# A seven-product (Strassen-Winograd) MLP pair on one core: four PSUM banks per set, P1 copied inside PSUM, sums reordered, Q4 sums on VectorE

## What is computed

```python
def _attn_ref(q, k, v, cap):                 # q, k, v: (2, 12, 448, 64)
    scores = cap * np.tanh(scale * (q @ k.T) / cap)
    attn = softmax(scores)
    return attn @ v
def _moe_ref(x, w_in, w_out):                # x: (896, 768), w_in: (768, 2048), w_out: (2048, 768)
    h = x @ w_in
    r = np.maximum(h, 0.0)
    return (r * r) @ w_out
def _moe2_ref(x, w_in, w_out):
    h = x @ w_in
    return (h / (1.0 + np.exp(-h))) @ w_out
reference = _moe2_ref(_moe_ref(_attn_ref(q, k, v, cap)))
```

## Time and profile before

| | us |
|---|---|
| median of 3 runs | 558.07 |
| the runs | 556.68, 558.07, 2859.89 |
| the profiled execution, its own time | 555.35 |
| its span (first to last instruction) | 553.1 |
| mean granted TensorE clock | 0.989 |

### The profile page before, as it was taken

How to read it: one execution, slowest core, us unless ns; L and a number is a source line. 1 busy time by engine, 2 the same in 40 slices (tenths; PEclk the granted TensorE clock), 3 DMA queues, 4 the chain that set the end, 5 groups by cost and what they waited for, 6 DMA issues and landing times.

```text
span 553.1 us, 7937 instructions
## 1 busy us (share of the span) xinstructions
...
## 2 busy tenths in 40 slices
...
GB/s 230 192 238 239 212 7 66 50 49 80 185 160 169 138 146 125 166 162 148 139 136 138 146 127 62 100 159 192 156 145 147 130 158 156 147 146 143 120 103 101
...
## 3 DMA queue, kind: packets, MB, share of 16 engines
...
...
## 4 chain that ended last, share of the span: by engine, by line
PE 47%; DVE 21%; ACT 15%; issue 8%; DMA 6%; ACTq 0%; DVEq 0%; POOL 0%; POOLq 0%
PE banks L678 12%; PE banks L679 12%; PE banks L680 12%; DVE g_all L1159 5%; ACT g_all L892 4%; PE banks L597 4%; DMA w_q<-w_raw 4%; DVE w_hl L1155 3%; PE banks L590 3%; DVE x_all L1212 2%; ACT work L878 2%; DVE work L1230 2%; ACT w_hl L842 2%; ACT work L885 2%; DVE y L1230 2%
## 5 line engine op out<-in xcount | busy, mean ns | idle before, releaser
L678 PE MATMUL banks<-g_all,w_hl 128*128 128x448 f32 (+1 forms) x339 | 126.3, 373 | 19.5 <-DVE y L1230 7.8
L678 PE MATMUL banks<-x_all,w_hl 128*128 128x448 f32 x342 | 124.9, 365 | 11.7 <-ACT work L859 8.5
L680 PE MATMUL banks<-x_all,w_hl 128*128 128x448 f32 x342 | 124.0, 363 | 0.0
L679 PE MATMUL banks<-g_all,w_hl 128*128 128x448 f32 (+1 forms) x339 | 124.0, 366 | 0.0
L679 PE MATMUL banks<-x_all,w_hl 128*128 128x448 f32 x342 | 123.8, 362 | 0.0
L680 PE MATMUL banks<-g_all,w_hl 128*128 128x448 f32 (+1 forms) x339 | 123.7, 365 | 0.0
L543 POOL DMA_DIRECT2D w_q<-w_raw x64 | 55.4, 973 | 148.2 <-DVE w_hl L1155 127.8
L842 ACT ACTIVATE w_hl<-w_q 128x384 fp32r<-128x384 f32 (+1 forms) x96 | 48.0, 500 | 75.2 <-PE banks L680 38.3
L678 PEld LDWEIGHTS banks<-g_all,w_hl 128*128 128x128 f32 x339 | 64.5, 190 | 34.2 <-issue 12.4
L842 ACT ACTIVATE w_hl<-w_raw 128x384 fp32r<-128x384 f32 (+1 forms) x128 | 63.5, 498 | 41.7 <-PE banks L680 41.4
L543 POOL DMA_DIRECT2D w_raw<-w_raw x32 | 28.5, 890 | 158.1 <-DMA w_raw<-in_moe_w_out_dram 90.6
...
## 6 DMA issues: line engine op xcount, KB each, us to landing
...
```

What stands on the lines that cost most here:

```text
L678: pe.matmul(dst, hi, mov_hi, start=start, stop=False, skip_group_check=onto)
L679: pe.matmul(dst, hi, mov_lo, start=False, stop=False, skip_group_check=onto)
L680: return pe.matmul(dst, lo, mov_hi, start=False, stop=stop, skip_group_check=onto)
```

## The change

The products keep their order. Post-additions are made over four banks A to D. ScalarE copies P1 (product 0) from bank A to bank C (`copy_p1`), where product 3 accumulates to C11. P5 (product 1, bank B) is copied by ScalarE to SBUF (`copy_p5`). VectorE adds bank A after product 2 and P5 into bank D (`make_d`), where product 5 accumulates to C12; product 4 accumulates in A, from which and P5 VectorE makes C22 (`make_22` in PAIR and first-stage GROUP sets; in others `ADD_P5` and `ADD_U3` onto y); product 6 accumulates in A to C21. C11, C12 and C21 of PAIR sets go through `shape` straight from their banks. In first-stage GROUP sets ScalarE copies C11, C12, C21 out; in later ones VectorE adds them to y. T2 and T4 of a PAIR set change tiles (work[0], t_sum). Layer 1's x sums go to work tiles in place of y. Q4 is added by VectorE in all seven-product sets (`add_q4`, before the T sums of the step n=0), and its DMA and the waits for it are gone; SP loads block (0,1) after split 6. The sums and low parts of x chunk 2 move from before set 2 into set 3, and the T1 parts of x to steps 5 and 6 of sets 2 to 4. The last product's two halves use banks A and B of the other half of PSUM. The orders on ScalarE and VectorE are rewritten by hand:

```diff
-    BANK_OF = (0, 1, 0, 2, 0, 1, 0)
-    ONTO = (2, 4, 5, 6)
-
+    BANK_A, BANK_B, BANK_C, BANK_D = range(4)
+    BANK_OF = (BANK_A, BANK_B, BANK_A, BANK_C, BANK_A, BANK_D, BANK_A)
+    ONTO = (2, 3, 4, 5, 6)
...
-               PAIR: (N_B11, N_B22, N_T1, N_T2, N_T3, N_B21, N_T4)}
+               PAIR: (N_B11, N_B22, N_T1, N_T2, N_B21, N_T3, N_T4)}
...
+            eng.wait_ge(s_g, g_no(ahead, {C11: N_T2, C12: N_T3, C22: N_B22, C21: N_B21}[block]))
+            eng.wait_ge(s_t, t_no(ahead, N_T3 if block == C22 else N_T4))
+            if s.kind == PAIR and s.layer == 1 and s.stage == 0 and s.i == 0 and block != C22:
+                eng.wait_ge(s_xo, xo_no(1, KP - 1, {C11: N_T2, C12: N_T3, C21: N_T4}[block]))
+            if block == C22 and sets[s.no - 1].kind == GROUP and sets[s.no - 1].stage > 0:
+                eng.wait_ge(s_take, take_no[sets[s.no - 1].no, ADD_P5])
...
-                    free = {(0, 0): 1, 0: 2, (0, 1): 4, (1, 0): 5, 1: 6, (1, 1): 7}
+                    free = {(0, 0): 1, 0: 2, (0, 1): 6 if q4_by_vector(ahead) else 4, (1, 0): 5, 1: 6, (1, 1): 7}
...
-                add_q4(ahead)
+                if not q4_by_vector(ahead):
+                    add_q4(ahead)
...
+                if n in (2, 3):
+                    pe.wait_ge(s_copy, copy_no[s.no, COPY_P1])
+                elif n in (4, 5):
+                    pe.wait_ge(s_take, take_no[s.no, MAKE_D])
                 else:
-                    pe.wait_ge(s_take, take_no[s.no, of])
+                    pe.wait_ge(s_take, take_no[s.no, MAKE_22 if MAKE_22 in taken_by_vector(s) else ADD_U3])
...
+                elif n == 5 and q4_by_vector(s):
+                    act.wait_ge(s_q4_v, q4_no(s))
...
+            def copy_p1(s):
+                act.wait_ge(s_prod, s.first + 1)
+                act.activation(bank(s, BANK_C), bank(s, BANK_A), ACT.Copy).then_inc(s_copy, 1)
+
+            def copy_p5(s):
+                act.wait_ge(s_prod, s.first + 2)
+                if s.kind == PAIR or s.stage > 0:
+                    work_free(act, s, C22)
+                elif s.layer == 0:
+                    act.wait_ge(s_xo, xo_no(0, s.i, N_T4))
+                act.activation(p5_tile(s), bank(s, BANK_B), ACT.Copy).then_inc(s_copy, 1)
...
+                elif block == C22:
+                    act.wait_ge(s_take, take_no[s.no, MAKE_22])
+                    src = acc(s, C22)
                     scale = -1.0
                 else:
-                    act.wait_ge(s_take, take_no[s.no, 3 + block])
-                    scale = -1.0 if block == C22 else 1.0
+                    n, bank_n = {C11: (3, BANK_C), C12: (5, BANK_D), C21: (6, BANK_A)}[block]
+                    act.wait_ge(s_prod, s.first + n + 1)
+                    src = bank(s, bank_n)
+                    scale = -1.0 if block == C21 else 1.0
+                if s.kind == PLAIN or block != C22:
+                    work_free(act, s, block)
...
-                    if n == 0 and 6 in copied_by_scalar(ahead):
-                        copy(ahead, 6)
+                    if n == 0 and ahead.kind == GROUP and ahead.stage == 0:
+                        copy_out(ahead, COPY_U4)
                     if n == 0 and ahead.kind == PAIR:
                         shape(ahead, C21)
...
-                    if n == 1 and 0 in copied_by_scalar(s):
-                        copy(s, 0)
-                    if n == 3 and 1 in copied_by_scalar(s):
-                        copy(s, 1)
-                        copy(s, 2)
-
-                    if n + 3 < NP:
+                    if n == 1:
+                        copy_p1(s)
+                    if n == 2:
+                        copy_p5(s)
+                    if n == 4 and first_out:
+                        copy_out(s, COPY_C)
+                    if n == 4 and s.kind == PAIR:
+                        shape(s, C11)
+                        square(s, C11)
+                    if n == 6 and first_out:
+                        copy_out(s, COPY_D)
+                    if n == 6 and s.kind == PAIR:
+                        shape(s, C12)
+                        square(s, C12)
+
+                    if n == 2 and q4_by_vector(s) or n < 2:
                         prod_high(s, n + 3)
-                    elif after:
-                        prod_high(after, n + 3 - NP)
-
-                    if s.kind == PAIR and n == 4:
-                        shape(s, C11)
+                    if n == 3 and q4_by_vector(s):
+                        prod_high(s, 6)
+                    if n == 4 and not q4_by_vector(s):
+                        prod_high(s, 6)
+                    if n >= 4 and after:
+                        prod_high(after, n - 4)
+
                     if s.kind == PAIR and n == 5:
-                        square(s, C11)
+                        g_high(s, N_B11)
                         shape(s, C22)
-                        g_high(s, N_B11)
+                        square(s, C22)
                     if s.kind == PAIR and n == 6:
-                        square(s, C22)
-                        shape(s, C12)
                         g_high(s, N_B22)
-                        square(s, C12)
...
                             g_high(ahead, N_T2)
+                            g_high(ahead, N_B21)
+                        if n == 2:
                             g_high(ahead, N_T3)
+                        if n == 3:
+                            g_high(ahead, N_T4)
...
                 if n == N_T1:
-                    wait(dve, s_t, 4 * s.pair)
+                    wait(dve, s_g, NP * s.pair)
+                    if s.layer == 1 and s.stage == 0 and s.i == 0:
+                        dve.wait_ge(s_xo, xo_no(1, KP - 1, N_T1))
                     dve.wait_ge(s_z, max(z_no(s, C11), z_no(s, C12)))
                     made = dve.tensor_tensor(t_sum[:, :], work[0][:, :], work[1][:, :], ALU.subtract)
                 elif n == N_T2:
                     dve.wait_ge(s_t, t_no(s, N_T1))
-                    dve.wait_ge(s_g, g_no(s, N_T1))
+                    dve.wait_ge(s_g, g_no(s, N_B11))
                     dve.wait_ge(s_z, z_no(s, C22))
-                    made = minus_both(t_sum[:, :], t_sum[:, :], work[3][:, :])
+                    made = minus_both(work[0][:, :], t_sum[:, :], work[3][:, :])
                 elif n == N_T3:
                     dve.wait_ge(s_t, t_no(s, N_T1))
                     dve.wait_ge(s_z, z_no(s, C22))
                     made = dve.tensor_tensor(work[1][:, :], work[3][:, :], work[1][:, :], ALU.subtract)
                 else:
                     dve.wait_ge(s_t, t_no(s, N_T2))
-                    dve.wait_ge(s_g, g_no(s, N_B21))
-                    made = minus_both(work[2][:, :], t_sum[:, :], work[2][:, :])
+                    dve.wait_ge(s_g, g_no(s, N_T1))
+                    dve.wait_ge(s_z, z_no(s, C21))
+                    made = minus_both(t_sum[:, :], work[0][:, :], work[2][:, :])
                 made.then_inc(s_t, 1)
...
+                else:
+                    dve.wait_ge(s_xo, xo_no(1, kk - 1, n))
+                if n == N_T1:
+                    dve.wait_ge(s_take, take_no[group.no, ADD_D])
+                    made = dve.tensor_tensor(t_sum[:, :], b11, b12, ALU.subtract)
+                elif n == N_T2:
+                    dve.wait_ge(s_xt, xt_no(1, kk, N_T1))
+                    made = minus_both(work[0][:, :], t_sum[:, :], b22)
+                elif n == N_T3:
+                    made = dve.tensor_tensor(work[1][:, :], b22, b12, ALU.subtract)
+                else:
+                    dve.wait_ge(s_xt, xt_no(1, kk, N_T2))
+                    dve.wait_ge(s_take, take_no[group.no, ADD_U4])
+                    made = minus_both(work[2][:, :], work[0][:, :], b21)
+                made.then_inc(s_xt, 1)
+
...
+            def add_q4(s):
+                dve.wait_ge(s_raw[s.no % 2][1], loads_of(s))
+                dve.wait_ge(s_w_lo, s.first + 3)
+                dve.tensor_tensor(q_block(s, 1), q_block(s, 1), raw_block(s, 0, 1), ALU.add).then_inc(s_q4_v, 1)
+
+            def make_d(s):
+
+                dve.wait_ge(s_prod, s.first + 3)
+                dve.wait_ge(s_copy, copy_no[s.no, COPY_P5])
+                dve.tensor_tensor(bank(s, BANK_D), bank(s, BANK_A), p5_tile(s), ALU.add).then_inc(s_take, 1)
+
+            def make_22(s):
+
+                dve.wait_ge(s_prod, s.first + 5)
+                dve.wait_ge(s_take, take_no[s.no, MAKE_D])
+                if s.kind == PAIR:
+                    dve.tensor_tensor(p5_tile(s), p5_tile(s), bank(s, BANK_A), ALU.add).then_inc(s_take, 1)
+                else:
+                    minus_both(p5_tile(s), p5_tile(s), bank(s, BANK_A)).then_inc(s_take, 1)
...
+            def add_out(s, what):
+
+                n, block, bank_n = {ADD_C: (3, C11, BANK_C), ADD_P5: (1, C22, None), ADD_U3: (4, C22, BANK_A),
+                                    ADD_D: (5, C12, BANK_D), ADD_U4: (6, C21, BANK_A),
+                                    LAST_U3: (4, C21, BANK_A)}[what]
```

(70 more changed lines are left out.)

259 lines of the change are left out of this document (126 added, 133 removed).

## The result

| kernel | runs | median us | lowest to highest | ratio to before, 95% interval |
|---|---|---|---|---|
| before | 4 | 557.51 | 556.68 to 558.07, and one of 2859.89 | 1 |
| changed | 4 | 535.44 | 534.91 to 539.03 | 0.962 [0.957, 0.967] |

The change makes the kernel 3.8% faster, 22.1 us between the medians; the forecast was 536.4. Nothing recorded explains the one run of 2859.89 us; it is left out of the ratio. The profiled execution of the changed kernel is its slowest, 539.03 us (span 536.6). Against the 555.35 of before (span 553.1) the two traces differ by only 16.5 us of span, and that is the difference they can explain.

A forecast was written before the change was run, and what follows sets the result against it. The bound was taken as chains between ScalarE and VectorE in strict program order. Window gains of 25.1 us less 3.4 for one clock dip gave 21.7, so 533.6 profiled and 536.4 us median; range 528 to 549.

The forecast's parts named there:

- P1 copied to bank C: 32 ScalarE copies between PSUM banks: 0.54 us each, chain 0.99 us, hidden inside product 1; no wait for T1's low part.
- The PAIR loops: PAIR sets in layer 0: product 2 loses 0.45 us from i=0 to i=1, 1.45 from i=1 to i=2.
- g(T1): T1 as operand of a GROUP set: its low part comes late, one wait of 2.65 us in sets 8 and 14.
- window 7: Seventh stage of TensorE's timeline, two-chunk sets: 2.6 of 5.4 us loss kept, 2.8 won.
- E(n): End of product n, counted as the start of the next matmul slot; copies waiting for it start 0.30 us later.
- Layer 1 (no squares): ScalarE's chain is four instructions shorter, copy_p1 ends 0.35 us before needed; PAIR windows 8 and 10 lose nothing.
- So I cost it at nothing: SP's load of block (0,1), about 1 us later (2 in two-chunk sets), is covered by 18 us (two-chunk 12).
- Entry: First window, sets 2 and 3: seven VectorE and three ScalarE instructions move to set 3; loss 4.6 instead of 10.0 us.
- rival D: VectorE becomes the queue, MAKE_D late in the 14 sets following a PAIR set: slower, 564 us; chance 0.07.
- Rival E: Q4's DMA was hidden anyway, its VectorE sum lengthens T1's chain: 6.6 us less gain, 543 us; chance 0.05.
- Rival A: No clock dip at all: 25.1 us won, 533.0 us; chance 0.20.
- rival B: Clock dips at sets 2, 8, 14 and 19 give 13.6 us back: 546.6 us; chance 0.08.

The follow-up runs named there:

- p1_copy_waits: Changed kernel with the P1 copy of PAIR sets again waiting for VectorE's low part of the previous pair's T1; 542.04 us, ratio 0.975.
- b22_first_only: Changed kernel with block (0,1)'s load released by split 4 and the Q4 sum, and ScalarE making B22's high part before C12; 527.24 us, ratio 0.947.
- t1_first: Changed kernel, block (0,1) released early; VectorE makes T1 before split 2 and Q4, its low part before T2; ScalarE makes B22's high part before C12; 526.45 us.
- release_01_early: Changed kernel with SP's load of block (0,1) waiting for split 4 and VectorE's Q4 sum instead of split 6; 533.28 us, ratio 0.959.
- changed_again: The changed kernel timed once more in the second batch with no edit; 535.45 us, ratio 0.960.
- entry_back: Changed kernel with the sums and low parts of x chunk 2 moved back from set 3 to before set 2; 537.87 us, ratio 0.966.
- q4_by_dma: Changed kernel with Q4 given back to the accumulating DMA, splits 5 and 6 one step later, block (0,1) released by split 4; 531.35 us, ratio 0.955.
- before_q4_by_vector: Kernel before with only Q4 moved to VectorE, in front of the T sums, and block (0,1) released by split 6; 562.98 us, ratio 1.009.

## Why the prediction was right, and where it was not

**The total.** 22.1 us between the medians against 21.7 forecast. Two misses inside it cancel, so that the totals agree so closely is luck. For the profiled execution I had 533.6 and it took 539.03 (again: 536.33), with 25.0 us of waits where I had 21.0, and 4.7 of clock where I had 3.4. And I carried 2.7 us over because the profiled execution of before lay that much under the median of its runs; after the change the profiled ones lie above it, by 3.6 and 0.9. One profile is a draw among the executions, and that offset should have been in the range and not in the sum.

**P1 copied to bank C: right.** 32 copies of 528 ns where I took 0.54 us, MAKE_D 630 and 632 ns for 0.62:

```profile
L894 ACT ACTIVATE banks<-banks 128x448 f32<-128x448 f32 x32 | 16.9, 528 | 10.7 <-PE banks L714 10.6
L1311 DVE TENSOR_TENSOR banks<-banks,work 128x448 f32<-128x448 f32 x26 | 16.4, 630 | 26.2 <-PE banks L714 26.2
...
L902 ACT ACTIVATE work<-banks 128x448 f32<-128x448 f32 x26 | 14.0, 540 | 9.3 <-PE banks L714 9.3
```

The Trainium skill ("ScalarE: Activation LUTs", "Step-by-step: what each stage is for") has PSUM as ScalarE's nearer destination. The rows agree in sign, 528 ns into a bank for 540 into SBUF (530 for the ReLU of L931, from a bank too): 2 to 12 ns, nothing for this kernel. The copy's value is that it waits for less: 6.6 us by p1_copy_waits, the largest part of the gain that was isolated.

**The PAIR loops: right to about 0.15 us.** 0.45 forecast and 0.58 and 0.57 measured in sets 6 and 12; 1.45 and 1.41 in 7 and 13; g(T1) of sets 8 and 14 2.65 and 2.54; T1 of set 17 1.6 and 1.50; the same wait in sets 25 and 31 0.85 and 0.86; window 7 2.6 and 2.5; window 10 none and none. The walk with E(n) + 0.30, the pitches and + 0.15 carried these. It failed in set 18, nothing forecast and 0.61 lost, at product 2: b22_first_only cuts it to 0.22 and t1_first to nothing, so it is the chain of sets 6 and 12, which "Layer 1 (no squares)" had declared short.

**"So I cost it at nothing": wrong.** The later load of (0,1) had, in the prediction, 12 us of cover in two-chunk sets. Behind it stand an accumulation of Q3 and one of Q2 that starts at its landing, and set 22 pays 2.0 us in one execution and 1.0 in the other, with a dip besides in the first. release_01_early shows the cause and changed_again, entry_back and p1_copy_waits that it recurs. I had counted the load's own landing and not the two sums behind it.

**Entry: right in sum, wrong inside.** 4.6 forecast, 5.0 kept. Set 2 lost 3.4 for 4.2. Set 3 lost 1.39 at MAKE_D for 0.4: MAKE_D starts at 139.92, and E(2)+0.30 was 138.27, so it came 1.65 us late and not "0.5 late". VectorE's timeline from set 3, the row before MAKE_D's run of instructions and the run's end:

```profile
135.45 0.43 DVE L1225 TENSOR_TENSOR w_hl<-w_q,w_hl 128x256 fp32r<-128x256 f32 x1 [0.97 <-ACT w_hl L882]
...
139.38 0.62 DVE L1299 TENSOR_TENSOR x_all<-y,x_all 128x448 fp32r<-128x448 f32 x1
139.92 0.63 DVE L1311 TENSOR_TENSOR banks<-banks,y 128x448 f32<-128x448 f32 x1
```

From 135.45 to 139.92 it waits for nothing: a wait of 0.97 us for ScalarE's split at the head of the row, which I had not walked, was carried through all of it, and makes 0.97 of the 1.65. In the other 31 sets TensorE never waits for MAKE_D: rival D did not come.

**Rival E, at 0.05, was right as to Q4.** I wrote that windows 1, 2 and 7 speak against it. They showed three sets where the DMA cost something (4, 5 and 21); a fourth that I named, set 2, was misread, for its split 5 started behind ScalarE's earlier instruction with no wait for a DMA. They did not show what the sum costs where T1's chain is late: q4_by_dma is 4.1 us faster than the changed kernel (1.9 faster than release_01_early, which shares its earlier load), before_q4_by_vector 5.2 us slower than before. The "35.0 us" of ScalarE's waits in the earlier trace rows misled me: q4_by_dma keeps eight of these waits, 10.4 us, and loses next to nothing by them.

**What the gain is made of.** It comes from the other parts: taking the copy's freedom away costs 6.6 us, and putting the entry back 2.4. The rest, among it the x sums in temporaries, C11 and C12 shaped straight from PSUM and the fewer bank waits in GROUP sets, was not tried by itself. If the parts simply add, 6.6 + 2.4 - 4.1 leaves some 17 of the 22.1 us to it. For that rest the evidence is the traces alone: the losses by window, and the bank waits that fell from 19.0 to 7.5 us.

**The clock: size close, places half right.** I counted one dip for 3.4 us and three came, of 1.6 us each, behind the two long waits that I named and behind set 22's, and none at 19. Rival A did not come: neither profiled execution of the changed kernel was without a dip. Nor did rival B, with its 13.6 us.
